# Diagonal entries of a decayed attention, formed in other places of four engines' programs, and idle turns of the unit matrix in another bank

## The chip, the cores and the metric

The kernel runs on one core of one Trainium2 chip, in one launch. The metric is the device time of that core in microseconds (us). Three runs of the kernel before gave 1082.68, 1085.60 and 1086.23 us, median 1085.6 us.

## The reference

Three parts follow one another. The first is a recurrent attention over 4 batches, 8 heads and 768 steps with head size 48; the other two are feed-forward layers of 3072 tokens. All is float32.

```python
for t in range(S):
    cur = einsum('bhd,bhe->bhde', u[None] * kt, vt)
    y[:, :, t] = einsum('bhd,bhde->bhe', rt, state + cur)
    state = wt[:, :, :, None] * state + einsum('bhd,bhe->bhde', kt, vt)
x  = (sigmoid(x @ w_gate) * (x @ w_val)) @ w_out      # 384 -> 1536 -> 384
h  = x @ w2_in                                        # 384 -> 2048
out = where(h > 0, h, exp(min(h, 0)) - 1) @ w2_out    # -> 384
```

## The kernel before, in words

The 768 steps are cut into six blocks of 128, and the four batches into two pairs. One block of one pair of batches is a "half" q, 0 to 11. In a half the lower triangle of the 128 by 128 scores A is filled level by level. Level li (L1 to L6) fills all off-diagonal squares of side 2^li: TensorE multiplies K and R of that level into a PSUM bank, and between two levels VectorE scales half of R (`next_level_r`, line 1148 in halves 0 and 1, lines 1152 and 1156 later) and GpSimd scales half of K (`next_level_k`, line 621) with products of the decay. The squares then move from PSUM into A: levels 1 to 3 by a predicated copy on VectorE (`masked_copies`, lines 1196 and 1201), levels 4 to 6 by copies on ScalarE (`score`, line 906, the line of the copy helper). The diagonal and the entries beside it inside each 2 by 2 square are the "near" entries. They come from sums over the head: GpSimd forms the products (`term`: rk at line 601, times u at line 608, r'k with the next step's r at line 596), VectorE sums them (`sum_own`, `sum_after`) and combines them to the tile `near` (`near_pairs`, lines 1173 and 1175), and `near_entries` (line 1180) writes them into A. KT turns the scaled K, Y (in half 0: Z and X) multiplies A with V, S forms the state. Each of these steps has two parts b, one for each batch.

PROGRAM is one list of steps that every engine walks through in the same order, each doing its share. Half 0 stands alone at the head of the list. From half 1 on the steps of a half are spread between thirds ("g", "v", "o": gate, value, output) of the first feed-forward layer of the tokens whose attention is done. ScalarE and VectorE also split each weight piece into a high and a low part (line 906 and line 1325); `SPLIT1` lays one piece behind each last third. SyncE loads piece x only when the split of piece x-4 (first pieces: x-8) has been counted (`d_wlo`), and its queue takes its transfers one by one in program order. TensorE multiplies a gate, value or output group only when the splits of its pieces are counted.

Each engine runs its own share strictly in order. So a wait in one step holds up all that is behind it on that engine. Halves 2 and later carry a state: their last scaling of R (level 6) goes into RP (line 1156) and is used in the second part of Y (line 816). Halves 4 and later take the levels in pairs: C1, D1, C3, D3, C5, D5 are steps in which ScalarE copies the unscaled halves of K and R (`a_copied`) and VectorE and GpSimd scale the originals, so that L1 and L2, L3 and L4, L5 and L6 follow each other on TensorE.

In half 0 nothing is there to fill TensorE's waits. It multiplies ("turns") the unit matrix in them (`turn_unit`, line 695), `IDLE[li]` times ahead of level li, into the bank that the level will write, and so behind that bank's release by the copies of two levels before. Banks 0 to 3 serve the levels of half 0, banks 5 to 7 the rest; bank 4 (`ACC + 2`) is first written by X.

The semaphores that matter: `d_mask` counts predicated copies, `a_score` counts the levels 4 to 6 copied by ScalarE (3 to a half), `d_near` the two steps of `near_pairs`, `d_diag` the written near entries (2 to a half), `d_r` and `p_k` the scalings. Y waits for `d_diag`, and GpSimd's `term` of the next half does too.

Of the kernel before, what the change touches and what calls it, by code (L numbers as in the profile page):

```python
# [13 lines left out]
def build(nc, r, k, v, w, u, w_gate, w_val, w_out, w2_in, w2_out, out):  # L14
# [17 lines left out]
    P = 128  # L32
# [195 lines left out]
    with ctx:  # L228
# [68 lines left out]
        a_copied = sem("a_copied")  # L297
# [369 lines left out]
        def _(pe):  # L667
# [23 lines left out]
            IDLE = {1: 6, 2: 0, 3: 10, 4: 10, 5: 10, 6: 5}  # L691
# [5 lines left out]
            def attention(q, name, b):  # L697
# [20 lines left out]
                elif name[0] == "L":  # L718
# [7 lines left out]
                    else:  # L726
                        heads = [ps[:, bank_of("a", q, name, e), :] for e in range(2)]
                        if b == 0:
                            for e in range(2):
                                bank_free("a", q, name, e)  # L730
                            if q == 0:
                                turn_unit(heads[0], IDLE[li])
# [40 lines left out]
                elif name == "Z":  # L773
# [6 lines left out]
                    pe.wait_ge(d_diag, 2 * q + b + 1)  # L780
# [123 lines left out]
        def _(act):  # L904
# [33 lines left out]
            def attention(q, name, b):  # L938
                hf = q % HALF
                if name[0] == "T" or name == "KT":  # L940
# [8 lines left out]
                    if x == 0 and quarters(q):  # L949
                        copy(R_DENSE[:, g, :], src).then_inc(a_evac, 1)  # L950
                    elif x == 0:
                        copy(R[0:HP, 0, g, :], src[0:HP])
                        copy(R[HP:P, 1, g, :], src[HP:P]).then_inc(a_evac, 1)
                    else:
                        copy((None, K, W, KM)[x][:, g, :], src).then_inc(a_evac, 1)
                elif name[0] == "C":
# [177 lines left out]
        def _(dve):  # L1134
# [32 lines left out]
            def near_pairs(q):  # L1167

                if q == 0:
                    dve.wait_ge(d_zero, 7)  # L1170
                dve.wait_ge(d_dots, q + 1)
                dve.wait_ge(d_shift, q + 1)
                nc.vector.tensor_scalar(near[:], dots[:, :, 1:3], even, None, ALU.mult).then_inc(d_near, 1)
                dve.wait_ge(d_near, 2 * q + 1)
# [3 lines left out]
            def near_entries(x, own):  # L1178
                pairs, n = slice(x * PR, (x + 1) * PR), own.stop - own.start
                return nc.vector.copy_predicated(  # L1180
                    A[own, pairs, :, own].rearrange("p g e (i j) -> p (g e) i j", j=2),
                    masks[own, 0, own.start // 2:own.stop // 2].bitcast(I32).unsqueeze(1).unsqueeze(3).to_broadcast([n, 2 * PR, n // 2, 2]),
                    near[own, 2 * x * PR:2 * (x + 1) * PR].unsqueeze(2).to_broadcast([n, 2 * PR, n // 2, 2]))
# [23 lines left out]
            def attention(q, name, b):  # L1207
# [12 lines left out]
                elif (name, b) == ("C3", 1):  # L1220
                    dve.wait_ge(s_att, count("a", q, "L1", 1))
                    masked_copies(q, 1)
                elif name[0] == "D":
# [10 lines left out]
                elif name[0] == "L" and not (paired(q) and int(name[1:]) % 2):  # L1234
# [8 lines left out]
                    if li < NL - 1 or q >= HALF:  # L1243
                        next_level_r(q, li, b)
                    if paired(q) and (li, b) == (4, 1):
                        masked_copies(q, 3)
                    elif not paired(q) and b == 1 and li < NM:
# [155 lines left out]
```

## Time and profile before

| | us |
|---|---|
| median of 3 runs | 1085.6 |
| lowest and highest | 1082.68, 1086.23 |
| profiled execution, its own time | 1086.84 |
| its span | 1085.1 |
| TensorE matmuls busy in the span | 1052.5 (97%) |
| VectorE, ScalarE, GpSimd busy | 613.9, 519.2, 252.4 |

The profiled execution is 1.2 us above the median and 0.6 us above the highest of the three runs; 1.7 us of its time lie outside the span. The mean granted clock of TensorE over the span is 0.989. In the page, a matmul's busy time is modelled and pipelined, a row of the timeline gives start, length, engine, line, tiles and count, and the bracket at its end the idle time before it and what ended that.

### The profile page before, as it was taken

The page shows a single profiled execution, that of the slowest core. Times are in us where ns is not written, and L with a number is a line of the kernel's source. Part 1 is how long each engine was busy: PE and PEld are TensorE (multiplying, and loading weights), DVE is VectorE, ACT ScalarE, POOL GpSimd, SP SyncE. Part 2 cuts the span into 40 slices and gives each one's busy share as a digit, 9 for nine tenths or more (in the row PEclk, how much of TensorE's full clock was granted, in tenths as well). Part 3 has the DMA queues.
Part 4 walks back from the last instruction along what each step waited for, and adds up shares of the span by engine and source line. Part 5 has one row for each costly group of instructions (what it writes and reads, how often), then busy time and mean ns, then how long its engine had stood idle before and what let it go on. Part 6 is the DMA issues. An engine that isn't in the chain of part 4 may idle for free.

```text
span 1085.1 us, 20897 instructions
## 1 busy us (share of the span) xinstructions
PE 1052.5 (97%) x8455; PEld 920.4 (85%) x8455; DVE 613.9 (57%) x918; ACT 519.2 (48%) x998; POOL 252.4 (23%) x255
## 2 busy tenths in 40 slices
PE   7888899999999999999999999999999999999998
PEld 6788888888888887888788888899999999989998
DVE  5686986768476847684867333534334343333433
ACT  2646435364546444545445333745445454544543
POOL 8231744354244424442443000000000000000000
PEclk7989999999999999999999999999999999999999
DMA  7554440404152214312200412201001010010000
GB/s 135 109 130 101 82 71 20 67 14 58 34 67 34 38 43 58 50 21 61 39 5 2 135 59 73 88 1 59 2 1 59 1 59 1 1 59 1 30 1 30
DMA packets 146463, 51.39 MB, mean 47 GB/s; under 512 B 116256, under 2 KB 144064, under 8 KB 146368
## 3 DMA queue, kind: packets, MB, share of 16 engines
q1 hardware_dynamic: 146368, 50.06, 22.1%
q8 instruction: 67, 1.10, 0.4%
q14 instruction: 28, 0.23, 0.1%
HBM read 39.52 MB, written 9.44 MB: 45 GB/s over the span
## 4 chain that ended last, share of the span: by engine, by line
PE 81%; DVE 10%; issue 4%; ACT 2%; DMA 1%; SPq 0%; POOL 0%; DVEq 0%; ACTq 0%; POOLq 0%
PE ps L850 22%; PE ps L885 18%; PE ps L877 18%; PE ps L860 10%; PE ps L716 3%; DVE A L1201 2%; PE ps L809 2%; DVE RKW L1152 2%; PE ps L816 2%; PE ps L760 2%; PE ps L764 1%; DVE hl L1303 1%; DVE work L1315 1%; PE ps L743 1%; PE ps L770 1%
## 5 line engine op out<-in xcount | busy, mean ns | idle before, releaser
L850 PE MATMUL ps<-xh,WS 128*128 128x512 f32 (+1 forms) x1008 | 250.1, 367 | 4.0 <-DVE WS L1325 2.8
L906 ACT ACTIVATE hh<-work 128x512 fp32r<-128x512 f32 (+1 forms) x180 | 108.6, 603 | 251.3 <-DVE work L1315 169.1
L850 PEld LDWEIGHTS ps<-xh,WS 128*128 128x128 f32 x1008 | 171.5, 189 | 31.8 <-DVE WS L1325 4.4
L885 PE MATMUL ps<-WS,hh 128*128 128x384 f32 x768 | 195.6, 336 | 0.6 <-DVE hl L1299 0.6
L621 POOL TENSOR_TENSOR RKW<-RKW,WL 128x256 f32<-128x256 f32 x144 | 133.2, 939 | 154.1 <-ACT work L906 67.7
L877 PE MATMUL ps<-xh,WS 128*128 128x512 f32 x576 | 161.5, 392 | 0.0
L1342 DVE SCALAR_TENSOR_TENSOR work<-work,ps 128x512 f32<-128x512 f32 x96 | 66.0, 687 | 165.4 <-ACT work L1093 165.4
L860 PE MATMUL ps<-hh,WS 128*128 128x512 f32 (+1 forms) x504 | 157.7, 368 | 0.8 <-DVE hl L1303 0.8
L885 PEld LDWEIGHTS ps<-WS,hh 128*128 128x128 f32 x768 | 139.8, 188 | 8.1 <-DVE hl L1299 1.1
L850 PE MATMUL ps<-xl,WS 128*128 128x512 f32 (+1 forms) x504 | 131.0, 368 | 0.0
L885 PE MATMUL ps<-WS,hl 128*128 128x384 f32 x384 | 128.8, 335 | 0.0
L877 PEld LDWEIGHTS ps<-xh,WS 128*128 128x128 f32 x576 | 107.0, 188 | 16.9
L1299 DVE TENSOR_TENSOR hl<-work,hh 128x512 fp32r<-128x512 f32 x96 | 66.5, 692 | 76.7 <-ACT hh L906 76.7
L1091 ACT ACTIVATE work<-ps 128x512 f32<-128x512 f32 x96 | 57.2, 595 | 109.1 <-PE ps L877 109.1
L860 PEld LDWEIGHTS ps<-hh,WS 128*128 128x128 f32 x504 | 92.3, 189 | 17.8 <-DVE hl L1303 3.0
L1152 DVE TENSOR_TENSOR RKW<-RKW,WL 128x512 f32<-128x512 f32 x100 | 82.2, 847 | 27.7 <-ACT work L906 16.6
L850 PEld LDWEIGHTS ps<-xl,WS 128*128 128x128 f32 x504 | 86.1, 189 | 13.8
L860 PE MATMUL ps<-hl,WS 128*128 128x512 f32 (+1 forms) x252 | 90.8, 360 | 0.0
L1048 ACT ACTIVATE work<-ps 128x512 f32<-128x512 f32 (+1 forms) x84 | 45.1, 537 | 87.1 <-PE ps L850 85.5
L1315 DVE TENSOR_TENSOR work<-work,ps 128x512 f32<-128x512 f32 (+1 forms) x84 | 51.3, 611 | 62.0 <-PE ps L850 49.5
L877 PE MATMUL ps<-xl,WS 128*128 128x512 f32 x288 | 81.5, 391 | 0.0
L1303 DVE TENSOR_TENSOR hl<-work,hh 128x512 fp32r<-128x512 f32 (+1 forms) x84 | 65.3, 777 | 18.1 <-ACT hh L906 17.3
(95 smaller groups left out, 1336.3 us busy)
## 6 DMA issues: line engine op xcount, KB each, us to landing
nat<-in_w_dram SPq DMA_DIRECT2D x24, 192.0 KB, 3.6
nat<-in_r_dram SPq DMA_DIRECT2D x24, 192.0 KB, 4.7
nat<-in_k_dram SPq DMA_DIRECT2D x24, 192.0 KB, 5.2
V<-in_v_dram SPq DMA_DIRECT2D x24, 192.0 KB, 4.2
x_scratch<-xs SPq DMA_DIRECT2D x12, 384.0 KB, 3.1
nat<-x_scratch SPq DMA_DIRECT2D x6, 768.0 KB, 5.9
out_dram<-A SPq DMA_DIRECT2D x5, 768.0 KB, 4.3
RKW<-in_moe_w_in_dram SPq DMA_DIRECT2D x16, 192.0 KB, 2.4
```

What stands on the lines that cost most here:

```text
L621: gp.tensor_tensor(Kb[:, :, :, 0, :], Kb[:, :, :, 0, :], Wb[:, :, :, 1].to_broadcast([P, PR, P // (2 * L), L]), ALU.mult).then_inc(p_k, 1)
L850: last = mm(val(m, j) if second else ps[:, GATE, t], gate_w(a, second, j, c), xp[b][:, c, t], start=(i == 0 and c == 0), stop=(i == 2 and ...
L860: last = mm(acc(m, i), down_w(a, j, i), parts_of(hp[b], m, j), start=(j == 0 and at == 0 and not (halved(m) and i == 1)), stop=(j == F1 - ...
L877: last = mm(ps[:, UP2 + j % 4, :], up2_w(a, j, c), xp[b][:, c, :], start=(i == 0 and c == 0), stop=(i == 2 and c == KC - 1))
L885: last = mm(ps[:, ACC2 + b, 0:HD], hp[ap][:, j % 2, b * P:(b + 1) * P], down2_w(wp, j), start=(j == 0 and i == 0), stop=(j == F2 - 1 and i ...
L906: return nc.scalar.activation(o, i, ACT.Copy)
L1091: nc.scalar.activation(sig, ps[:, UP2 + j % 4, :], ACT.Relu, scale=-1.0).then_inc(a_relu, 1)
L1152: last = tt(Rb, Rb, Wb.unsqueeze(1).unsqueeze(3).to_broadcast([P, 2, n, L]), ALU.mult)
L1299: tt(hl[:, j % 2, :], h[:], f32(hh[:, j % 2, :]), ALU.subtract).then_inc(d_lo, 1)
L1303: tt(parts_of(hl, m, j), h[:, turn(m, j)], f32(parts_of(hh, m, j)), ALU.subtract).then_inc(d_lo, 1)
L1315: tt(h[:, turn(m, j)], sig[:, turn(m, j)], val(m, j), ALU.mult).then_inc(d_h, 1)
L1342: nc.vector.scalar_tensor_tensor(h, sig, -1.0, ps[:, UP2 + j % 4, :], ALU.add, ALU.max).then_inc(d_elu, 1)
```

## The change

There are six edits. (1) `IDLE` is now 6, 4, 8, 8, 6, 4 turns for levels 1 to 6 (it was 6, 0, 10, 10, 10, 5); the turns go to bank 4 and stand ahead of the wait for the level's own banks. (2) In half 0, the first step of `near_pairs` (the product with `even`) moves from VectorE to ScalarE, at L5 b=0, and the second stands behind VectorE's scaling at L5 b=1. (3) In half 0 the near entries are written as four squares of 32 by 32, all heads in each, and wait for the ScalarE copy of level 4 alone; before, they were two squares of 64 by 64 for each batch and waited for level 5 too. Z waits for all of them. (4) In half 1 `near_pairs` and the near entries stand behind `sum_after` in L6 b=1; before, in KT. (5) In halves 2 to 11 the last scaling of R of b=1 moves from L6 b=1 to behind the near entries of b=1 in KT. (6) In halves 4 to 11 the predicated copies of level 3 move from L4 b=1 to C5 b=0.

```diff
@@ TensorE
-            IDLE = {1: 6, 2: 0, 3: 10, 4: 10, 5: 10, 6: 5}
+            IDLE = {1: 6, 2: 4, 3: 8, 4: 8, 5: 6, 6: 4}
...
                         if b == 0:
+                            if q == 0:
+                                turn_unit(ps[:, ACC + 2, :], IDLE[li])
                             for e in range(2):
                                 bank_free("a", q, name, e)
-                            if q == 0:
-                                turn_unit(heads[0], IDLE[li])
...
-                    pe.wait_ge(d_diag, 2 * q + b + 1)       (Z only)
+                    pe.wait_ge(d_diag, 2 * (q + 1))
@@ ScalarE
+                elif (q, name, b) == (0, "L5", 0):
+                    act.wait_ge(d_zero, 7)
+                    act.wait_ge(d_dots, q + 1)
+                    act.wait_ge(d_shift, q + 1)
+                    nc.scalar.activation(near[:], dots[:, :, 1:3], ACT.Copy, scale=even).then_inc(a_near, 1)
@@ VectorE
             def near_pairs(q):
+                dve.wait_ge(d_dots, q + 1)
+                dve.wait_ge(d_shift, q + 1)
                 if q == 0:
                     dve.wait_ge(d_zero, 7)
...
+                    dve.wait_ge(a_near, 1)
+                else:
+                    nc.vector.tensor_scalar(near[:], dots[:, :, 1:3], even, None, ALU.mult).then_inc(d_near, 1)
+                    dve.wait_ge(d_near, 2 * q)
...
+            def near_of_batch(q, b):
+                dve.wait_ge(a_score, (NL - NM) * (q + 1))
+                dve.wait_ge(d_near, 2 * q + 1)
+                near_entries(slice(b * PR, (b + 1) * PR), slice(0, P)).then_inc(d_diag, 1)
...
+                elif (name, b) == ("C5", 0):
+                    dve.wait_ge(s_att, count("a", q, "L3", 1))
+                    masked_copies(q, 3)
...
-                    if li < NL - 1 or q >= HALF:
+                    if li < NL - 1 or q >= HALF and b == 0:
                         next_level_r(q, li, b)
-                    if paired(q) and (li, b) == (4, 1):
-                        masked_copies(q, 3)
...
-                    if name == "L5" and b == 0 and q != 1 and not paired(q):
+                    if name == "L5" and b == int(q == 0) and q != 1 and not paired(q):
                         near_pairs(q)
                     if (q, name, b) == (0, "L6", 1):
...
-                        dve.wait_ge(a_score, (NL - NM) * (q + 1) - 1)
-                        dve.wait_ge(d_near, 2 * (q + 1))
-                        for x in range(U):
-                            for own in (slice(0, HP), slice(HP, P)):
-                                last = near_entries(x, own)
-                            last.then_inc(d_diag, 1)
+                        dve.wait_ge(a_score, (NL - NM) * q + 1)
+                        dve.wait_ge(d_near, 2 * q + 1)
+                        for x in range(0, P, P // 4):
+                            last = near_entries(slice(0, G), slice(x, x + P // 4))
+                            if x >= HP:
+                                last.then_inc(d_diag, 1)
                 elif name == "KT" and q > 0:
-                    if (q, b) == (1, 0):
-                        near_pairs(q)
-                    dve.wait_ge(a_score, (NL - NM) * (q + 1))
-                    dve.wait_ge(d_near, 2 * (q + 1))
-                    near_entries(b, slice(0, P)).then_inc(d_diag, 1)
+                    if q > 1:
+                        near_of_batch(q, b)
+                    if q > 1 and b == 1:
+                        next_level_r(q, NL - 1, b)
...
                     sum_after(q)
+                    if q == 1:
+                        near_pairs(q)
+                        for x in range(U):
+                            near_of_batch(q, x)
```

## Rows read from the trace of the kernel before

**Rows 1.** Waits of TensorE: line, releaser, total us, times, longest us
```profile
PE ps L809 <- DVE A L1180: 5.4, 3, 2.4
...
PE ps L770 <- DVE RKW L1152: 3.5, 5, 0.8
PE ps L850 <- DVE WS L1325: 2.8, 1, 2.8
```
**Rows 2.** Timeline of TensorE in half 0: start, length, what
```profile
1.84 3.25 PE L695 MATMUL ps<-ident 128*128 128x128 f32 x14 [1.84 <-POOL ident L568]
...
11.17 0.82 PE L695 MATMUL ps<-ident 128*128 128x128 f32 x6
...
17.38 2.37 PE L695 MATMUL ps<-ident 128*128 128x128 f32 x10 [1.29 <-DVE A L1196]
19.68 1.93 PE L743 MATMUL ps<-RKW 64*64 64x32 f32 x64
...
30.61 1.22 PE L748 MATMUL ps<-RKW 64*64 64x64 f32 x32
...
35.27 0.43 PE L782 MATMUL ps<-A,V 128*48 128x128 f32 x4 [0.65 <-DVE A L1180]
```
**Rows 3.** Timeline of VectorE in half 0
```profile
17.27 1.50 DVE L1148 TENSOR_TENSOR RKW<-RKW,WL 128x256 f32<-128x256 f32 x2
18.80 1.57 DVE L1196 COPY_PREDICATED A<-masks,ps 64x256 f32<-64x256 int32 x4
...
31.95 3.27 DVE L1180 COPY_PREDICATED A<-masks,near 64x512 f32<-64x512 int32 x4 [0.85 <-ACT A L906]
```
**Rows 4.** Timeline of GpSimd in half 0
```profile
18.45 2.14 POOL L608 TENSOR_TENSOR prod<-prod,ub 128x384 f32<-128x384 f32 x2
...
20.87 1.73 POOL L621 TENSOR_TENSOR RKW<-RKW,WL 128x256 f32<-128x256 f32 x2 [0.28 <-PE ps L743]
```
**Rows 5.** Windows at 30 and at 57 us: stretch, its us, busy of five engines, TensorE's clock, DMA
```profile
30.00:31.00 1.00, 1.00 (x17) 0.83 (x19) 0.96 (x3) 0.79 (x3) 0.72 (x2) 1.00 1.11 167
57.00:64.00 7.00, 6.02 (x82) 5.73 (x83) 5.87 (x15) 1.77 (x5) 1.76 (x2) 0.52 0.66 147
```
**Rows 6.** Timeline of SyncE's queue behind half 0
```profile
33.76 1.73 SPq L450 DMA_DIRECT2D shift<-in_r_dram  x2
37.74 0.35 SPq L477 DMA_DIRECT2D work<-in_moe_w_out_dram  x1
```
**Rows 7.** Timeline of TensorE at the end of half 1
```profile
91.45 0.52 PE L850 MATMUL ps<-xh,WS 128*128 128x256 f32 x3
...
94.69 3.62 PE L809 MATMUL ps<-A,V 128*48 128x128 f32 x32 [2.37 <-DVE A L1180]
```
**Rows 8.** Timeline of VectorE at the end of half 1
```profile
88.75 0.94 DVE L1161 TENSOR_REDUCE dots<-shift 128x16 f32<-128x768 f32 x1
90.31 0.56 DVE L1325 TENSOR_TENSOR WS<-work,WS 128x384 fp32r<-128x384 f32 x1 [0.61 <-ACT WS L906]
...
93.23 2.50 DVE L1180 COPY_PREDICATED A<-masks,near 128x1024 f32<-128x1024 int32 x2
```
**Rows 9.** Timeline of TensorE in Y of halves 2 and 3
```profile
138.07 1.08 PE L809 MATMUL ps<-A,V 128*48 128x128 f32 x16 [1.32 <-DVE A L1180]
...
173.75 1.08 PE L809 MATMUL ps<-A,V 128*48 128x128 f32 x16 [1.72 <-DVE A L1180]
```
**Rows 10.** Timeline of VectorE ahead of Y of half 2
```profile
133.15 3.12 DVE L1156 TENSOR_TENSOR RKW<-RKW,WL 64x256 f32<-64x256 f32 x4
```
**Rows 11.** Half 4: TensorE's second part of level 6
```profile
221.07 0.69 PE L770 MATMUL ps<-RKW 128*64 128x64 f32 x16 [0.80 <-DVE RKW L1152]
```
**Rows 12.** Half 4: VectorE's copies of level 3
```profile
214.49 1.46 DVE L1201 COPY_PREDICATED A<-masks,ps 64x512 f32<-64x512 int32 x2
215.98 0.69 DVE L1315 TENSOR_TENSOR work<-work,ps 128x512 f32<-128x512 f32 x1
```
**Rows 13.** Half 4: ScalarE ahead of C5
```profile
216.78 0.63 ACT L906 ACTIVATE hh<-work 128x512 fp32r<-128x512 f32 x1 [6.84 <-DVE work L1315]
```

More of the change, by code:

```diff
@@ L296, in build @@
         p_const, p_masks, p_zero = sem("p_const"), sem("p_masks"), sem("p_zero")
-        a_copied = sem("a_copied")
+        a_copied, a_near = sem("a_copied"), sem("a_near")
         p_shift, p_diag, p_k, p_sw = (sem(n) for n in ("p_shift", "p_diag", "p_k", "p_sw"))
@@ L779, in attention @@
                         pe.wait_ge(v_loaded[hf], 32)
-                    pe.wait_ge(d_diag, 2 * q + b + 1)
+                    pe.wait_ge(d_diag, 2 * (q + 1))
                     for e in range(2):
@@ L1167, in near_pairs, with near_entries @@
             def near_pairs(q):
+                dve.wait_ge(d_dots, q + 1)
+                dve.wait_ge(d_shift, q + 1)
                 if q == 0:
                     dve.wait_ge(d_zero, 7)
[L1171 to L1174, printed above, removed]
+                    dve.wait_ge(a_near, 1)
+                else:
+                    nc.vector.tensor_scalar(near[:], dots[:, :, 1:3], even, None, ALU.mult).then_inc(d_near, 1)
+                    dve.wait_ge(d_near, 2 * q)
                 nc.vector.scalar_tensor_tensor(near[:], dots[:, :, 0:2], odd, near[:], ALU.mult, ALU.add
                                                ).then_inc(d_near, 1)
-            def near_entries(x, own):
-                pairs, n = slice(x * PR, (x + 1) * PR), own.stop - own.start
+            def near_entries(pairs, own):
+                m, n = 2 * (pairs.stop - pairs.start), own.stop - own.start
                 return nc.vector.copy_predicated(
                     A[own, pairs, :, own].rearrange("p g e (i j) -> p (g e) i j", j=2),
-                    masks[own, 0, own.start // 2:own.stop // 2].bitcast(I32).unsqueeze(1).unsqueeze(3).to_broadcast([n, 2 * PR, n // 2, 2]),
-                    near[own, 2 * x * PR:2 * (x + 1) * PR].unsqueeze(2).to_broadcast([n, 2 * PR, n // 2, 2]))
+                    masks[own, 0, own.start // 2:own.stop // 2].bitcast(I32).unsqueeze(1).unsqueeze(3).to_broadcast([n, m, n // 2, 2]),
+                    near[own, 2 * pairs.start:2 * pairs.stop].unsqueeze(2).to_broadcast([n, m, n // 2, 2]))
+            def near_of_batch(q, b):
+                dve.wait_ge(a_score, (NL - NM) * (q + 1))
+                dve.wait_ge(d_near, 2 * q + 1)
+                near_entries(slice(b * PR, (b + 1) * PR), slice(0, P)).then_inc(d_diag, 1)
             def masked_copies(q, li):
@@ L1242, in attention @@
                         dve.wait_ge(p_zero, 4)
-                    if li < NL - 1 or q >= HALF:
+                    if li < NL - 1 or q >= HALF and b == 0:
                         next_level_r(q, li, b)
-                    if paired(q) and (li, b) == (4, 1):
-                        masked_copies(q, 3)
-                    elif not paired(q) and b == 1 and li < NM:
+                    if not paired(q) and b == 1 and li < NM:
                         masked_copies(q, li)
-                    if name == "L5" and b == 0 and q != 1 and not paired(q):
+                    if name == "L5" and b == int(q == 0) and q != 1 and not paired(q):
                         near_pairs(q)
```

## Prediction, made before the changed kernel was built or run

> **What bounds the kernel now.** I read five views in this order: the busy times, TensorE's waits, the timelines of half 0, the granted clock, and then the places at which the waits lie. TensorE is busy 97% of the span (the table above), so beside half 0 a gain can only come out of what TensorE waits for. There the largest wait is for the near entries: 5.4 us in three places, the Y of halves 1, 2 and 3 [rows 1, 7, 9]. The next that the change touches is 3.5 us at level 6, behind the scaling of R: four times 0.8 (the even halves from 4 on) and 0.3 once in half 2 [rows 1, 11]. From half 4 on no Y waits for near entries.
>
> Half 0 is a chain. From 17.4 us on TensorE's own work is its bound: ten turns take 2.37 us, the 64 matmuls of a level 1.93 us, the next turns start at once, and this 4.2 us step repeats for levels 3, 4 and 5 (matmuls at 19.7, 23.9, 28.1) [rows 2]. The clock explains the size: a turn at 17.4 us takes 237 ns, as one of the very first 14 does (232 ns), while one of the six at 11.2 us takes 137; from 30 us on full clock is granted [rows 2, 5]. So the clock rose behind the first turns, fell behind levels 1 and 2, and levels 3 to 5 ran at half (1.2 GHz). At the end another chain decides: near entries from 31.95 to 35.22 us, started by a ScalarE copy, and Z behind them at 35.27 us [rows 2, 3].
>
> **Half 0, part by part.** (a) Turns. The total goes from 41 to 36; four of them now fill the pause between levels 1 and 2 (about 0.4 us, at full clock) and cost nothing there. The turns ahead of level 3 no longer wait for the predicated copy that ended at 17.24 us, but start when level 2 ends, at 16.1. I take first the case that the clock falls as before. Eight turns at 235 ns are 1.9 us, so TensorE is free at 18.0. VectorE's first scaling of level 2 is done at 17.27 + 0.75 = 18.0 [rows 3]; matmuls 18.0 to 20.0 (before to 21.6, 1.6 early). Eight turns to 21.9. GpSimd is now next: its product with u ends at 18.45 + 2.14 = 20.6, its scaling of K takes 1.73/2 = 0.87 for each batch, so the first batch is ready at 21.5 [rows 4]: just hidden. Level 4 runs 21.9 to 23.8, 2.0 early. Six turns (1.4 us) to 25.2, level 5 to 27.1, 2.9 early. Four turns to 28.0, level 6 (1.22 us for 32 matmuls in the part that ran at full clock [rows 2], up to 1.9 at half) to 29.9; GpSimd's scaling (0.87), KT and the four turns ahead of Z bring Z to about 32.3 us, against 35.27: 3.0 us.
>
> (b) If instead the clock stays full, the turns are short and GpSimd and VectorE bind: GpSimd's level 3 ends at 22.3, r'k (1.8, as long as its rk) at 24.1, level 4 at 25.6, so level 5 ends near 26.2 and VectorE's last scaling at 26.9. Z then follows the near entries.
>
> (c) Near entries. VectorE writes four squares of 32 partitions by 512 elements in place of four of 64 by 512 [rows 3]. No row has 32 partitions; I take the same 0.82 us each (3.27/4), because the rows with 64x512 and 128x1024 go by elements, not partitions (0.82 and 1.25 [rows 3, 8]). What changes is the start. It no longer waits for the copy of level 5, and the first step of near on ScalarE (a small operation, 0.2 to 0.6 us) lies in a wait of that engine for level 5; without that cover it would cost those 0.2 to 0.6. Start 27.9 in case (a), 27.3 in (b); end 31.2 or 30.5. In (a) this is below TensorE's own 32.3, in (b) it sets Z at 30.6: 4.7 us. Nothing decides between (a) and (b), since levels 1 and 2 with their pauses were followed by the fall, and the change fills one pause and removes the 1.29 us one. I take the middle, **3.8 us**.
>
> A rule of the Trainium skill speaks against (b): the page "TensorE: Matmul & The Clock Gate", section "Part 4: PE-mode transpose", says that transposes do not count as activity for the full clock. The turns are transposes. By that rule filling pauses would not hold the clock and (a) holds, 3.0 us. The trace speaks against the rule: nothing but transposes and turns had run before the six turns at 11.2 us, and these ran at the short time [rows 2].
>
> Does the gain of half 0 last? X, the next transposes and the weight splits follow Z in a chain. SyncE's queue is busy until 33.76 + 1.73 = 35.5 us, then idle until the first split is counted, 37.7 [rows 6]; its next piece is first used at 51 us, so 2.2 us earlier is enough and 3.8 is no conflict.
>
> **Half 1.** Before: sums until 89.7, split of piece 30 at 90.31 to 90.87, near entries 93.23 to 95.73; Y at 94.69 after 2.37 us idle, and then 3.62 us for 32 matmuls, where 16 take 1.08 elsewhere [rows 7, 8, 9]: the clock had fallen. After: near (0.5) and its entries (2.5) run 89.7 to 92.7. What is queued behind them is the split of piece 30, now done at 93.3, for which TensorE's gate group of 91.45 waits; then Y directly, at 94.2. So only **0.5 us** of the 2.37 come back, since one wait takes the place of the other. But the pause is then 1.8 us with matmuls close on both sides. Pauses of 1.32 and 1.72 us in halves 2 and 3 left Y's first 16 matmuls at 1.08 [rows 9], 2.37 did not. 1.8 is nearest to 1.72: I take the clock as kept, **1.6 us** (3.62 less 2 x 1.0), with 0 as the other end.
>
> **Halves 2 and 3.** VectorE's four scalings take 3.12 from 133.15 [rows 10]. Now only two (1.56) come first, then a gate product of 256 columns (about 0.4, from the 0.69 of 512 [rows 12]), then the entries of b=0 (1.25 [rows 8]): done at about 136.4, where TensorE is ready at 136.75. Y starts without a wait. The moved scaling ends at 136.4 + 1.25 + 1.56 = 139.2; the fourth part of Y, which needs it, starts three parts later, each 0.9 to 1.08 us, at 139.4 or later. So all **1.3 us** come back. In half 3 the same sum puts the entries at 172.0 and the scaling at 174.75 against 174.65: **1.6** of 1.72. GpSimd's products for the next half, released by these entries, start 1.5 us sooner and now run beside the moved scaling; if they slow it by half, that is 0.4 us in each (low end 0.9 and 1.2).
>
> **Halves 4 to 11.** The copies of level 3 (1.46 us) move behind the gate product that they delayed: product, then hh on ScalarE, which had idled 6.84 us for it, then C5, D5, level 6 [rows 12, 13]. The inputs of that product were there at 213.5, the copies started at 214.49. So D5 comes about 1.4 us sooner, and the wait of 0.80 goes [rows 11]. What is late next: GpSimd's scaling, which has 0.4 us in hand. In the odd halves TensorE waits for none of this. **4 x 0.8 = 3.2 us** (low end 2.4). The moved scaling of R would end at about 229.4 us in half 4, and the fourth part of Y, which needs it, starts at 232.4; half 5 gives 276.3 and 279.4. With 3 us of slack it costs nothing.
>
> **Sum.** 3.8 + 0.5 + 1.6 + 1.3 + 1.6 + 3.2 = 12.0 us. Against the profiled execution's 1086.84 that is 1074.8. Its three timed runs have a median 1.2 us lower, but part of that may be the clock's luck in half 0, which the change touches; I stay at **1075 us**. With all low ends (3.0, 0.3, 0, 0.9, 1.2, 2.4) the gain is 7.8, the time 1079; with all high ends (4.7, 0.7, 1.7, 1.3, 1.7, 3.2) it is 13.3, 1073.5.
>
> **Rivals.** (A) The gain of half 0 is absorbed between 53 and 97 us, where SyncE issues weight pieces one behind the other. If this queue is bound by something that does not move with half 0, 3.8 us are lost: 1078.6. For it: Y of half 1 waited in a stretch in which splits waited for data. Against it: the queue's loads wait for splits, which move along, and its next issue was idle until 37.74 [rows 6].
>
> (B) More than forecast. The 2.8 us wait of line 850 ahead of 58 us [rows 1] also let the clock fall: half for nearly all of 57 to 64 us (mean 0.52) [rows 5], some 6.8 us whose work would take 3.4 at full. If the wait gets shorter with the shift, these 3.4 us go too: 1071.4.
>
> (C) The turns do not do what they are for: fewer of them, in other places, leave the clock at half for longer in half 0 (into X, as much as the 3.8 gained), half 1 falls as before (1.6), and one more stretch like the one of 57 to 64 us comes in (3.4): 1083.6, no change that can be told.
>
> (D) Slower. In halves 4 to 11 the near entries wait for ScalarE's copy of level 6 and now hold the last scaling of R behind them. This decides once the scaling ends more than its 3 us of slack late; from there each of eight halves pays its whole 1.56, 12.5 us, and halves 2 and 3 lose their 2.9: 1090.2. Against it: in half 4 the copy of level 6 ends at 224.3 us and the entries began only at 225.5.
>
> **How the numbers follow.** Forecast 0.55, A 0.18, B 0.12, C 0.09, D 0.06. Likeliest is the forecast, 1075. The range takes in forecast, A and B with the unknown ends: 1069.5 to 1082; C and D (0.15) lie outside. About 0.3% (3.3 us) is what a measurement of this kernel can tell from no change: faster than 1082.3 are forecast, A and B, 0.85; within 0.3% C, 0.09; slower D, 0.06.
>
> **What would show it.** In the changed profile: turns at about 16.1 us without the wait for line 1196; Z near 31 to 32.5 and X some 3 to 5 us sooner; in half 1 a wait of line 850 for a split in place of the one of line 809; no wait of line 809 for line 1180 in halves 2 and 3; no 0.8 at line 770. The prediction is wrong if line 816 waits for line 1156, if the idle of TensorE between 53 and 97 us grows by what half 0 gave, or if the half clock behind 16 us lasts longer than before.

## The result, and the profile after

| | before | after |
|---|---|---|
| median, us | 1082.77 | 1077.35 |
| lowest and highest | 1082.03, 1086.23 | 1076.22, 1077.94 |
| runs | 5 | 5 |
| profiled execution, its own time | 1086.84 | 1077.94 |
| its span | 1085.1 | 1076.2 |
| mean granted clock of TensorE | 0.989 | 0.993 |

The ratio is 0.9945 [0.9925, 0.9964]: 5.4 us less of medians. A second measurement of the same two kernels gave 1076.08 against 1082.63 and 0.9941 [0.9928, 0.9954]: 6.6 us of medians. The forecast of 1075.0 was 2.4 and 1.1 us too low, and inside its range. But it was made of 12.0 us counted from an execution that itself stood 4.1 us above the median measured here: the gain measured is half of the sum, and the terms don't stand as they were priced. That is what the experiments are about.

In the changed kernel the near entries are line 1188 (they were 1180), the scalings of R lines 1154, 1158 and 1162 (1148, 1152, 1156), the split of a weight piece line 1344 (1325). First, what TensorE waits for after the change: line, releaser, total us, times, longest us.

```profile
PE ps L850 <- DVE WS L1344: 4.8, 2, 2.8
PE ps L764 <- DVE RKW L1158: 3.9, 6, 1.2
PE ps L743 <- POOL RKW L621: 2.7, 3, 1.1
...
PE ps L816 <- DVE RKW L1162: 1.6, 2, 0.9
...
PE ps L782 <- DVE A L1188: 1.1, 1, 1.1
...
PE ps L809 <- DVE A L1188: 0.5, 1, 0.5
```

Beside [rows 1]: of the 5.4 us behind line 1180 at line 809, 0.5 us is left (in half 3), and of the 3.5 us at line 770, 0.3. In their place stand 2.0 us more for splits (line 850) and 1.6 us for the scaling of R that was moved (line 816). The timeline of TensorE in half 0 and that of the near entries on VectorE (start, length, line, and in the bracket the idle time before and its releaser):

```profile
16.02 1.09 PE L695 MATMUL ps<-ident 128*128 128x128 f32 x8
18.23 1.27 PE L743 MATMUL ps<-RKW 64*64 64x32 f32 x64 [1.11 <-DVE RKW L1154]
...
21.52 1.46 PE L743 MATMUL ps<-RKW 64*64 64x32 f32 x64 [1.00 <-POOL RKW L621]
...
31.66 0.65 PE L782 MATMUL ps<-A,V 128*48 128x128 f32 x8 [1.07 <-DVE A L1188]
...
33.32 0.68 PE L791 MATMUL ps<-y,SW 128*128 128x128 f32 x4 [0.29 <-ACT y L906]
```
```profile
27.82 3.69 DVE L1188 COPY_PREDICATED A<-masks,near 32x512 f32<-32x512 int32 x4
```

A turn takes 136 ns (1.09/8), where those of [rows 2] at 17.38 took 237. So the clock stayed full, and a level waits for GpSimd and VectorE, as case (b) had it. Z now runs in one piece from 31.66; before, its first batch started at 34.20 and its second, the row at 35.27 in [rows 2], only there. X (line 791) starts at 33.32 in place of 36.72.

I then laid the two traces of TensorE over each other, matmul by matmul, and read how much sooner the changed kernel is at several places, named by the time of before:

| at, us of before | what lies behind | after | after, second execution |
|---|---|---|---|
| 36.7 | half 0, at X | 3.4 | 3.7 |
| 82.6 | | 1.1 | 3.4 |
| 98.95 | half 1 | 3.8 | 5.7 |
| 147 | half 2 | 4.0 | 5.9 |
| 182 | half 3 | 4.5 | 6.3 |
| 1070 | halves 4 to 11, second layer | 9.9 | 11.9 |

Of the 9.9 us at the last matmul the span shows 8.9, since the last transfer landed 3.5 us behind the last copy and not 2.4.

### The profile page after: what moved, and what is told of

It is laid out like the page before. It is cut to its first block, busy times and chain, and to the rows that moved or that the text cites. A ratio compares the mean times of both kernels' runs of the same rounds, so it can differ in the third digit from the quotient of the medians.

```text
span 1076.2 us, 20906 instructions
## 1 busy us (share of the span) xinstructions
PE 1047.3 (97%) x8450; PEld 915.9 (85%) x8450; DVE 626.5 (58%) x917; ACT 520.9 (48%) x999; POOL 251.8 (23%) x255
## 4 chain that ended last, share of the span: by engine, by line
PE 87%; DVE 7%; issue 2%; ACT 1%; DMA 1%; SPq 0%; POOL 0%; DVEq 0%; POOLq 0%; ACTq 0%
PE ps L850 25%; PE ps L885 19%; PE ps L877 18%; PE ps L860 12%; PE ps L716 3%; PE ps L760 2%; PE ps L764 2%; PE ps L809 2%; PE ps L816 1%; DVE A L1209 1%; PE ps L770 1%; DVE work L1334 1%; DVE A L1188 1%; DVE RKW L1154 1%; DVE A L1214 1%
## 5 line engine op out<-in xcount | busy, mean ns | idle before, releaser
L621 POOL TENSOR_TENSOR RKW<-RKW,WL 128x256 f32<-128x256 f32 x144 | 130.4, 921 | 151.7 <-ACT work L906 57.4
L1322 DVE TENSOR_TENSOR hl<-work,hh 128x512 fp32r<-128x512 f32 (+1 forms) x84 | 67.5, 804 | 15.1 <-ACT hh L906 14.1
```

The lines of the kernel that those rows point to most:

```text
L621: gp.tensor_tensor(Kb[:, :, :, 0, :], Kb[:, :, :, 0, :], Wb[:, :, :, 1].to_broadcast([P, PR, P // (2 * L), L]), ALU.mult).then_inc(p_k, 1)
L1322: tt(parts_of(hl, m, j), h[:, turn(m, j)], f32(parts_of(hh, m, j)), ALU.subtract).then_inc(d_lo, 1)
```

## The experiments

Each kernel is measured against runs of the kernel before on the same chip, in between its own. The medians of these were 1083.2 (turns, near0, half1, copies3), 1082.63 (after_again, head, order_r, pool_later) and 1084.3 us (late1, x_late, lean, turn_place). A ratio is against its own median of before.

### The edits one by one

**turns**: edit (1) alone.

```diff
-            IDLE = {1: 6, 2: 0, 3: 10, 4: 10, 5: 10, 6: 5}
+            IDLE = {1: 6, 2: 4, 3: 8, 4: 8, 5: 6, 6: 4}
...
                         if b == 0:
+                            if q == 0:
+                                turn_unit(ps[:, ACC + 2, :], IDLE[li])
                             for e in range(2):
                                 bank_free("a", q, name, e)
-                            if q == 0:
-                                turn_unit(heads[0], IDLE[li])
```

> Only the turns of half 0 are changed (their counts, bank 4, ahead of the bank's wait). Theory T (a ledger read from the profile of the changed kernel against that of before): the turns held the clock at full through half 0, and the near entries then only have to follow. Z would still wait for the copy of level 5 and the old near chain. I expect full clock throughout 12 to 32 us, level 5 done near 26.3 instead of 30 us, and X 2.5 to 3.4 us earlier than before (36.7); total 2 to 4 us shorter where nothing later takes it back. Rival R1: levels stay at half clock without the rest, X less than 1.5 us earlier, total within 1 us. Rival R2: the weight stage from 50 to 90 us takes the gain back, total within 1 us although X is early.

Measured 1081.9, ratio 0.9988 [0.9973, 1.0004]: 1.3 us, and not shown apart from nothing. X started at 33.05, 3.7 us sooner than in the profiled execution of before, and yet the total was not 2 to 4 us shorter, as I had expected.

**near0**: edits (2) and (3) alone.

```diff
-                    pe.wait_ge(d_diag, 2 * q + b + 1)
+                    pe.wait_ge(d_diag, 2 * (q + 1))
...
+                    nc.scalar.activation(near[:], dots[:, :, 1:3], ACT.Copy, scale=even).then_inc(a_near, 1)
...
-                        dve.wait_ge(a_score, (NL - NM) * (q + 1) - 1)
...
-                        for x in range(U):
-                            for own in (slice(0, HP), slice(HP, P)):
-                                last = near_entries(x, own)
...
+                        dve.wait_ge(a_score, (NL - NM) * q + 1)
...
+                        for x in range(0, P, P // 4):
+                            last = near_entries(slice(0, G), slice(x, x + P // 4))
```

> Only the near entries of half 0 are changed (first step on ScalarE, squares of 32 by 32, without the wait for level 5). Theory T: TensorE's own turns at half clock bind levels 3 to 5, so the near entries start at most some 1 us sooner (level 5's scalings end at 30.7 us as before, entries from about 31.2) and X is 0.3 to 1.0 us earlier; total 0 to 1 us shorter. Rival R3: the near entries were the bound of half 0: X 2.5 us or more earlier.

Measured 1084.25, ratio 1.0010 [0.9991, 1.0029]: no difference that can be told. X started at 34.65.

**half1**: edit (4) alone.

```diff
                 elif name == "KT" and q > 0:
-                    if (q, b) == (1, 0):
-                        near_pairs(q)
...
+                    if q > 1:
+                        near_of_batch(q, b)
...
                     sum_after(q)
+                    if q == 1:
+                        near_pairs(q)
+                        for x in range(U):
+                            near_of_batch(q, x)
```

> Only the near entries of half 1 move from KT to behind the last sum in level 6. Theory T (by my sum): Y starts 0.5 us earlier, because the split of piece 30 is now behind the entries, and Y runs at full clock, 2.0 instead of 3.6 us: total about 2 us shorter. Rival R4: the pause ahead of Y just moves to the gate group in front of it and the clock falls all the same: within 0.5 us.

Measured 1084.19, ratio 1.0012 [0.9995, 1.0028]: no difference that can be told, and not the 2 us that I had expected. The timeline of TensorE at the end of half 1 shows the wait in its new place:

```profile
91.27 0.62 PE L850 MATMUL ps<-xh,WS 128*128 128x256 f32 x3 [1.94 <-DVE WS L1331]
91.73 0.51 PE L850 MATMUL ps<-xl,WS 128*128 128x256 f32 x3
92.17 1.95 PE L809 MATMUL ps<-A,V 128*48 128x128 f32 x32
```

**copies3**: edit (6) alone.

```diff
+                elif (name, b) == ("C5", 0):
+                    dve.wait_ge(s_att, count("a", q, "L3", 1))
+                    masked_copies(q, 3)
...
-                    if paired(q) and (li, b) == (4, 1):
-                        masked_copies(q, 3)
-                    elif not paired(q) and b == 1 and li < NM:
+                    if not paired(q) and b == 1 and li < NM:
                         masked_copies(q, li)
```

> Only the predicated copies of level 3 in halves 4 to 11 move behind the gate product. Theory T: the wait of 0.80 us at line 770 goes in halves 4, 6, 8 and 10, and something of 0.3 us in a pair of halves more (the ledger shows 1.3 us for each pair): total 3.2 to 5.3 us shorter. Rival R5: the 0.3 us belong to the moved scaling of R: 3.2 us.

Measured 1077.51, ratio 0.9943 [0.9925, 0.9961]: 5.7 us. One edit of six gives about what the whole change was measured to give. Levels 5 and 6 of half 4, in the timeline of TensorE, of the kernel before and then of copies3:

```profile
218.33 1.47 PE L760 MATMUL ps<-work,RKW 128*64 128x64 f32 x32
219.63 0.64 PE L770 MATMUL ps<-RKW 128*64 128x64 f32 x16
...
221.69 0.97 PE L850 MATMUL ps<-xl,WS 128*128 128x512 f32 x3
```
```profile
215.02 1.15 PE L760 MATMUL ps<-work,RKW 128*64 128x64 f32 x32
216.00 1.10 PE L770 MATMUL ps<-RKW 128*64 128x64 f32 x32
217.04 0.97 PE L850 MATMUL ps<-xl,WS 128*128 128x512 f32 x3
```

From the first matmul of level 5 to the next gate product it was 3.36 us (221.69 - 218.33) and is 2.02: 1.34 in each of four halves, 5.4 us. Only 0.8 of it was a wait that the view of the waits named [rows 11]. Another 0.3 lay inside the row of line 760, whose 32 matmuls took 1.47 and now take 1.15, and 0.2 in the row of line 770.

**order_r**: edit (5) alone.

```diff
-                    if li < NL - 1 or q >= HALF:
+                    if li < NL - 1 or q >= HALF and b == 0:
                         next_level_r(q, li, b)
...
+                    if q > 1 and b == 1:
+                        next_level_r(q, NL - 1, b)
```

> Only the last scaling of R of b=1 moves behind the near entries of b=1, halves 2 to 11. My sum: 2.9 us shorter, all in halves 2 and 3. Theory C (contention): GpSimd's products of the next half, released by the near entries, now run beside the moved scaling, which takes 2.4 us instead of 1.6; line 816 waits for it 0.9 and 0.6 us, and 0.7 us in all are left of the 2.9; halves 4 to 11 lose nothing. Total 0 to 1 us shorter.

Measured 1081.97, ratio 0.9992 [0.9981, 1.0004]. This kernel has the half 0 of before, instruction for instruction, and yet X started at 32.88, sooner than in the changed kernel. That says more of half 0 than of edit (5).

### Half 0: what the clock does by itself

The windows from 14 to 31 us of five executions: the stretch, its us, busy time of TensorE (matmuls, weight loads), VectorE, ScalarE, GpSimd, then TensorE's granted clock, the DMA share and GB/s. In this order: before, copies3, order_r (all three with the old half 0), turns, after.

```profile
14.00:31.00 17.00, 15.07 (x312) 13.48 (x307) 12.90 (x25) 2.93 (x11) 13.05 (x14) 0.60 0.59 130
```
```profile
14.00:31.00 17.00, 14.30 (x335) 12.62 (x333) 14.79 (x27) 4.96 (x16) 14.34 (x16) 0.80 0.57 127
```
```profile
14.00:31.00 17.00, 12.78 (x339) 10.75 (x339) 16.27 (x29) 5.90 (x18) 13.98 (x16) 1.00 0.53 124
```
```profile
14.00:31.00 17.00, 12.86 (x342) 10.47 (x334) 16.14 (x29) 5.74 (x18) 14.07 (x16) 1.00 0.53 126
```
```profile
14.00:31.00 17.00, 12.33 (x337) 10.19 (x330) 16.40 (x28) 6.46 (x19) 14.40 (x16) 1.00 0.54 128
```

The first three have the same instructions in half 0, and yet the clock differs. The changed kernel's two executions differ as well, with no half clock and 3.4 us of it in half 0. So how long the half clock lasts in half 0 depends on the execution too, and a single trace doesn't show what a kernel costs. With the turns in their old place it lasted 13.7 us (before), 10.2 (near0), 10.2 (half1), 6.8 (copies3) and 0 (order_r), and X started at 36.72, 34.65, 34.77, 34.00 and 32.88, in the mean at 34.6. The profiled execution of before was the worst of the five. In order_r, at full clock, the ten turns behind the 1.28 us wait are short, and the near entries start just as soon as in the changed kernel:

```profile
17.23 1.28 PE L695 MATMUL ps<-ident 128*128 128x128 f32 x10 [1.28 <-DVE A L1196]
...
32.88 0.68 PE L791 MATMUL ps<-y,SW 128*128 128x128 f32 x4 [0.30 <-ACT y L906]
```
```profile
28.11 3.26 DVE L1180 COPY_PREDICATED A<-masks,near 64x512 f32<-64x512 int32 x4 [0.35 <-ACT A L906]
```

In the changed kernel they start 0.3 us sooner (27.82), but take 3.69 us in place of 3.26, and Z now waits for all of them. The four squares of 32 by 32, which I had taken at 0.82 us each, took 1.17, 1.02, 0.72 and 0.72. The first two ran beside GpSimd's scalings of K, as its timeline in the changed kernel shows:

```profile
27.79 1.65 POOL L621 TENSOR_TENSOR RKW<-RKW,WL 128x256 f32<-128x256 f32 x2 [0.54 <-PE ps L748]
```

The 0.82 us were such a mean too: of the four copies of 64 by 512 in [rows 3] the one beside a scaling of K took 1.03, the others 0.72 to 0.73. The near edits of half 0 gain nothing here, at either clock.

**head**: edits (1) to (3) together, that is the diffs of turns and near0.

> Half 0 as in the change (turns and near entries), all later halves as before. Theory L: 1.2 to 2.5 us shorter than before, a little more than the turns alone (1.3), since only both together let Z start behind entries at 31.5 us. Rival A: within 0.5 us of before. My prediction's sum: 3.8 us shorter.

Measured 1081.57, ratio 0.9992 [0.9983, 1.0001], 1.1 us of medians; X at 33.26. No more than turns alone (33.05).

**turn_place**: the turns in their new place and bank, but their old counts, 41 in all (the diff of turns without its first two lines).

> Before with its old counts of turns, but in bank 4 and ahead of the waits for the level's banks. It tells the place from the counts (turns: both, 1.3 us shorter). If the removed pause ahead of level 3 holds the clock, half 0 is at full clock throughout and the total 1 us or so shorter, as with both. If the four turns between levels 1 and 2 do, a half-clock stretch is seen behind 15 us and the total is that of before, within 0.5 us.

Measured 1082.82, ratio 0.9984 [0.9965, 1.0003]; X at 33.00, and granted full clock from 7.5 to 55.2 us. X is as early as in turns, so the new place and bank are enough, and the smaller number adds nothing that shows. Of nine executions with the new place, seven showed no half clock in half 0 and two (the second of the changed kernel, and x_late below) 3.4 us of it; apart from x_late, in which X is held on purpose, X started between 32.83 and 33.32, in the mean at 33.1. Against 34.6 that is 1.5 us, which agrees with the medians of turns, head and turn_place (1.3, 1.1 and 1.5 us less), though each of their intervals just takes in no change. It is a gain in certainty: what the old place had in its best execution, the new one has in nearly all.

**x_late**: the changed kernel with 26 turns of the unit matrix ahead of X, to see whether a shift of half 0 reaches the end.

```diff
+                    turn_unit(ps[:, GATE, :], 26)
                     pe.wait_ge(a_put, 1)
```

> The changed kernel with 26 more turns ahead of X, which makes X and all behind it 2.5 to 3 us later (116 ns each at full clock, 0.3 us of them hidden). It is the probe for rival A. If the weight stage takes up what half 0 gains or loses, the total stays within 1 us of the changed kernel (1076 to 1077.4). If it passes it on, as theory L says, the total is 2.5 to 3 us longer: 1078.6 to 1080.4.

Measured 1080.69, ratio 0.9965 [0.9946, 0.9985]. X started at 35.52, 2.2 and 2.5 us later than in the two executions of the changed kernel. The ratio is higher by 0.0020 and 0.0024 than theirs, which is 2.2 to 2.6 us; the medians differ by 3.3 and 4.6. The timeline shows the turns and X behind them:

```profile
32.63 3.06 PE L695 MATMUL ps<-ident 128*128 128x128 f32 x26
35.52 0.61 PE L792 MATMUL ps<-y,SW 128*128 128x128 f32 x4
```

The intervals of these ratios overlap, so they alone don't settle it. The fourteen traces say the same: from X to the matmul that before has at 98.95 TensorE took 62.2 us in before, where X was latest (36.72), 61.1 in x_late (35.52), and 60.0 to 62.1 in the twelve others (32.83 to 34.77). If the stage of the weight pieces absorbed a shift, it would have been shortest where X was latest. So the shift comes through, as far as these runs can tell.

### Halves 1 to 3: who takes the place of the wait

**after_again**: the changed kernel once more, without an edit, beside the kernels that are compared with it.

> The changed kernel once more, with runs of before between. Four single edits have been timed: turns -1.3 us, near entries of half 0 +1, of half 1 +1 (both within noise of none), copies of level 3 -5.7. Theory L (luck of one trace): the profiled execution of before had a long half-clock stretch in half 0 that most of its runs don't have, so the 3.4 us read there are mostly not the change's. Expected: ratio 0.993 to 0.996 (5 to 7 us). In the profile X at 33 to 34 us and no half clock in half 0. Rival A (the weight stage takes the head's gain back): the same total, but then the shift against before shrinks between 50 and 98 us in this look too.

Measured 1076.08, 0.9941 [0.9928, 0.9954], with X at 33.03. It shows half 1 a second time. The first time the gain fell from 3.0 us (at 73) to 1.1 at 82.6. There a split took 2.06 us, where one takes 0.56 alone, and TensorE waited 2.02 us for it; behind that wait the clock was at half from 82.0 to 88.9. The rows of VectorE and GpSimd of after, then VectorE's of after_again:

```profile
78.94 2.06 DVE L1344 TENSOR_TENSOR WS<-work,WS 128x384 fp32r<-128x384 f32 x1 [0.60 <-ACT WS L906]
```
```profile
78.78 1.80 POOL L596 TENSOR_TENSOR shift<-shift,nat 128x768 f32<-128x768 f32 x1
```
```profile
77.66 0.98 DVE L1344 TENSOR_TENSOR WS<-work,WS 128x384 fp32r<-128x384 f32 x1 [0.50 <-ACT WS L906]
```

GpSimd's product starts 0.16 us ahead of the split and ends at 80.58, the split at 81.00, 0.42 us later and so within less than the 0.56 that it takes alone: as if nearly all of it had waited for the product. The Trainium skill has this as a rule (page "SBUF — State Buffer", section "SBUF: two separate sides"): a GpSimd operation that reads SBUF and a VectorE operation with two inputs in SBUF share a pair of ports, and whoever starts first has it for its whole instruction. The trace agrees: the split took 2.06 us, 1.50 more than alone. An operation with one of its inputs in PSUM was not held up. In half 5 of before VectorE's product of line 1315 ran within one of GpSimd's, of 275.15 to 277.00 us, and took the 0.69 us that it takes alone:

```profile
276.23 0.69 DVE L1315 TENSOR_TENSOR work<-work,ps 128x512 f32<-128x512 f32 x1 [1.21 <-issue]
```

**pool_later**: the changed kernel, but GpSimd's products for the next half wait for the last scaling of R, not for the near entries ahead of it.

```diff
-                        pool.wait_ge(d_diag, 2 * (q + 1))
+                        pool.wait_ge(d_r, scaled(q, NL - 1, 1))
```

> The changed kernel, but GpSimd's products of the next half wait for the moved scaling of R instead of the near entries. Theory C: without GpSimd beside it the scaling of b=1 takes 0.8 to 1.6 us instead of 2.4, the waits of line 816 (0.9 and 0.6 us) fall to 0.3 or less each, and the time is 0.8 to 1.5 us below the changed kernel of the same call. Rival P (position): the scaling is late because it stands behind the entries, whatever GpSimd does: the waits stay above 0.5 us each and the time is the changed kernel's.

Measured 1075.25, ratio 0.9931 [0.9919, 0.9944], 0.8 us below after_again, though the two intervals overlap; what the wait did is read from the traces. VectorE's timeline in half 2, of after and of pool_later:

```profile
134.20 2.36 DVE L1162 TENSOR_TENSOR RKW<-RKW,WL 64x256 f32<-64x256 f32 x2
136.59 1.93 DVE L1322 TENSOR_TENSOR hl<-work,hh 128x256 fp32r<-128x256 f32 x1
```
```profile
133.60 0.85 DVE L1162 TENSOR_TENSOR RKW<-RKW,WL 64x256 f32<-64x256 f32 x2
134.48 0.42 DVE L1322 TENSOR_TENSOR hl<-work,hh 128x256 fp32r<-128x256 f32 x1
```

The two scalings cost 2.36 us beside GpSimd and 0.85 alone, and the next instruction 1.93 against 0.42: 1.5 us for each product of 1.8 to 2.0 us met. One by one, the first scaling (134.20) had started 0.24 us ahead of GpSimd's product and took 0.40; the second took 1.95 and ended at 136.56, 0.28 us behind the product's end. What it did to TensorE, after first and then pool_later:

```profile
136.70 1.08 PE L816 MATMUL ps<-RKW,ST 128*48 128x128 f32 x16 [0.91 <-DVE RKW L1162]
```
```profile
135.02 1.04 PE L816 MATMUL ps<-RKW,ST 128*48 128x128 f32 x16
```

By the shift against before, halves 2 and 3 gave 0.7 us in after, 0.8 in order_r and 2.2 in pool_later.

**late1**: pool_later, and half 1's predicated copies of level 1 moved behind the split of the piece that TensorE waits for ahead of 58 us [rows 1].

```diff
-                    if not paired(q) and b == 1 and li < NM:
+                    if not paired(q) and b == 1 and li < NM and (q, li) != (1, 1):
...
+                if step == ("d", 0, "g", 2, 2):
+                    dve.wait_ge(s_att, count("a", 1, "L1", 1))
+                    masked_copies(1, 1)
```

> The changed kernel with GpSimd's products behind the moved scaling (as pool_later), and the predicated copies of level 1 in half 1 moved from L1 b=1 to behind the split of weight piece 10, which they delayed. Theory V (VectorE is the bound between 50 and 58 us): the 2.8 us wait of line 850 at 55 us, which every look shows, falls below 1 us, the half-clock stretch behind it goes, and at 98 us TensorE is 2 us or more ahead of pool_later; total 2 to 4 us below pool_later's 1075.3, so about 1072. Rival Q (the queue of weight pieces is the bound from 50 to 97 us): the wait goes but comes back at other pieces, total within 1 us of pool_later.

Measured 1075.89, ratio 0.9915 [0.9896, 0.9934]; against another before this can't be told from pool_later's 0.9931, and it isn't the 2 to 4 us less that I had expected. The wait of 2.81 us ahead of 58 us went, but the same edit made another. In the timeline of TensorE in late1:

```profile
54.33 1.40 PE L743 MATMUL ps<-RKW 64*64 64x32 f32 x64 [1.62 <-issue]
...
67.11 0.62 PE L850 MATMUL ps<-xh,WS 128*128 128x256 f32 x3 [1.03 <-DVE WS L1344]
...
70.17 0.62 PE L850 MATMUL ps<-xh,WS 128*128 128x256 f32 x3 [1.74 <-DVE WS L1344]
```

and that of VectorE, with the copies that were moved:

```profile
51.60 2.63 DVE L1209 COPY_PREDICATED A<-masks,ps 64x256 f32<-64x256 int32 x4
```

The view names no releaser for the 1.62 us, but this is level 2, which writes a bank that the copies of level 1 free, and it starts 0.10 us behind their end at 54.23. At 58.0 us of before's time late1 was 6.2 us ahead of before and pool_later 3.6; at 60.0 it was 5.5 and 4.5, at 73 it was 2.7 and 2.5. So of the 2.6 us that late1 had over pool_later, 1.6 went to this wait. The last 0.8 went by 73, where both wait for splits: late1 for 1.03 and 1.74 us, pool_later for 2.21 at 70.40 us.

SyncE issues the transfers of the pieces back to back in this stage, one 0.47 us behind the other, with a long one now and then. In after:

```profile
83.74 0.44 SPq L475 DMA_DIRECT2D work<-in_moe_w_gate_dram  x1
84.22 1.86 SPq L474 DMA_DIRECT2D work<-in_moe_w_val_dram  x1
86.13 0.44 SPq L475 DMA_DIRECT2D work<-in_moe_w_val_dram  x1
86.61 0.42 SPq L474 DMA_DIRECT2D work<-in_moe_w_val_dram  x1
87.08 0.44 SPq L475 DMA_DIRECT2D work<-in_moe_w_val_dram  x1
```

That this queue sets the pace of the stage is what these rows suggest; no run changed the queue alone.

### A version without the near edits

**lean**: the kernel before with turns (edit 1), order_r (edit 5) with the wait of pool_later, and copies3 (edit 6). The near edits (2), (3) and (4) are left out.

> Before plus the turns, the moved scaling of R with GpSimd's products behind it, and the copies of level 3; the near entries of halves 0 and 1 stay as before. Reading of the runs so far: the near edits of halves 0 and 1 give nothing (a run of half 0 with unchanged near entries at full clock had X at 32.9 us, the changed kernel 33.3). Then lean is within 0.7 us of pool_later: 1074.6 to 1076. If they do give something, lean is 1 us or more above it.

Measured 1074.89 (1074.23 to 1076.35), ratio 0.9909 [0.9889, 0.9928]: the lowest ratio and median of all, though its interval overlaps those of late1 and pool_later and just meets those of the changed kernel. Y of half 1 starts without a wait in it, with the near entries in their old place.

## Why the time came near the forecast and the terms did not hold

| term | predicted, us | what the runs show |
|---|---|---|
| half 0 | 3.8 | 1.1 to 1.5 by medians, all by edit (1), no interval clear of nothing |
| half 1 | 0.5 + 1.6 | nothing that can be told (half1: 1.0012) |
| halves 2 and 3 | 1.3 + 1.6 | 0.7 by the shift |
| halves 4 to 11 | 4 x 0.8 = 3.2 | 4 x 1.34 = 5.4; by medians 5.7 |
| sum | 12.0 | 7.4 on average; measured 5.4 and 6.6 |

The sum was not right. The time came within 2.4 us of the forecast because a sum of twice the gain was taken from an execution that lay 4.1 us too high, and that is luck. The mean of the two measurements is 6.0, so some 1.4 us of the sum of parts stay unexplained; both intervals (3.9 to 8.1 and 5.0 to 7.8 us) take that sum in. The parts can't be known better than that: the runs of before alone lay between 1080.4 and 1092.0, and their four medians between 1082.6 and 1084.3.

**Half 0: the step that failed was to take the profiled execution's clock for the kernel's.** The working (a turn of 237 ns, so half clock) read the trace rightly, and X came 3.4 us sooner than in that trace, near the 3.8 forecast. But I saw that the execution lay above all of its three timed runs, wrote that part of it might be the clock's luck, and changed nothing for it in the sum. It was a large part: 2.1 us of X's start (36.72 against a mean of 34.6). Of my cases (a) and (b) it was (b), and Z came at 31.66 and not 30.6: the near entries began at 27.8 (27.3 forecast) and took 3.69, not 3.27, since two of them met GpSimd's scalings of K. The 35.27 that I measured Z against was its second batch alone; at X, where both kernels are at one point, the gain is 3.4. That the near edits bring half 0 nothing I had not seen; at full clock the old near entries are not late.

The rule of the Trainium skill that I weighed, that transposes don't count as activity for the full clock ("TensorE: Matmul & The Clock Gate", "Part 4: PE-mode transpose"), now has more against it than [rows 2]. turn_place moves nothing but turns of the unit matrix into other places and another bank, and the half clock of 6.8 to 13.7 us, which four of five old executions had, was absent.

**Half 1.** "One wait takes the place of the other" was right, and line 850 took over, as forecast. Both prices were wrong. The 2.37 us wait and the 3.62 us Y at half clock [rows 7] are again this one execution's: in the seven others that have half 1's near entries in their old place (lean, turns, near0, copies3, turn_place, order_r, head) the wait was 0, 0.30, 0.56, 1.19, 1.22, 1.25 and 1.49 us, and Y took 2.16 to 2.28. There was no fallen clock in their Y to win back. What remains is a Y of 1.96 in place of 2.27, 0.3 us, and against it a wait of 1.8 to 2.0 for the split that the near entries delay, in half1, after_again, pool_later and late1.

**Halves 2 and 3.** The wait of line 809 went in half 2; in half 3, 0.49 us of the 1.72 stayed (0.47 to 0.53 in all seven executions with edit (5)). There the two scalings of b=0 took 1.81 us and not 1.56, and the first near entries 1.50 and not 1.25. The step that failed is the price of the company. The sum took the moved scaling at 1.56 us for two, with 0.4 us more only at the low end, and the near entries at 1.25 each. In half 2 of after the two scalings took 2.36. The near entries took 3.34 and not 2.5, since in their new place they met GpSimd's products of line 651. From the start of the first scaling to the end of the moved one that is 7.1 us where I had counted 6.0, with 0.2 us in hand. It was written down what would show this wrong, a wait of line 816 for the scaling, and there it is: 0.91 and 0.64 us. With the products released later (pool_later) 2.2 of the 2.9 us came, and the wait in half 3 is most of what is missing.

**Halves 4 to 11.** The mechanism was right and the size too small, since I priced only the wait that the view names. The stall began one row sooner, inside the 32 matmuls of line 760, where a group's length hides it.

**Rivals.** A (absorbed by the weight stage) gave 1078.6; the first median lay 1.3 us from it, nearer than to the forecast, the second 2.5, further off. Its mechanism has the traces against it: the stage from X on was no shorter where X was late (x_late). Whether it holds for gains made inside the stage stays open: late1 lost 0.8 of its last 1.0 us there, in one execution. B (a shorter wait ahead of 58 us): that wait is 2.81 us before and after, it moved with half 0, and the half clock behind it lasted 6.8 us both times. C: the turns did hold the clock. D: line 816 waited for the scaling in halves 2 and 3 alone, so in none of halves 4 to 11. What stays open is which part of the 37 to 99 us stretch is luck: the gain between X and the end of half 1 was 0.2 to 2.2 us in the seven kernels without edit (4), and 0.4 to 2.2 in the six executions with it, so these traces say nothing of the edit. The timed runs of half1 leave between 0.5 us less and 3.0 us more open, and so not the 2.1 us that were forecast.

## What to carry to other kernels

Before you price a stall at half clock, look at a second execution of the same kernel; where the profiled one lies above the timed runs, the clock's stretches are the first thing to suspect, and a stall that they caused is no gain to be had. For an engine that only fills pauses, put the filling ahead of its waits, not behind. When you move an operation of VectorE, ask which GpSimd instruction its new neighbours release, and let that wait for the operation, and don't take its time alone for its time there. Price a stall from the start of one fixed instruction to the start of the next, not by the idle time alone.

## What the runs showed of the chip

- The granted clock in one and the same half 0 was at half for 0, 6.8 and 13.7 us in three executions (order_r, copies3, before). The two ends differ by 3.8 us at X.
- VectorE operations with two inputs in SBUF didn't share time with a GpSimd product that had begun before them, they stood still until it ended: 0.42 became 1.95 us, 0.42 became 1.93, and 0.56 became 2.06. A scaling that had begun 0.24 us ahead of the product took 0.40, and one with an input in PSUM took its 0.69.
- The predicated copies of near entries, whose two inputs lie in SBUF, were held up as well: 128 by 1024 elements took 1.28 to 1.35 us alone and up to 1.96 beside a GpSimd product.
- Alone, a predicated copy of 32 partitions by 512 elements took 0.72 us and one of 64 by 512 took 0.73: half the partitions save nothing.
